# Convolving two blocks in idle PSUM banks, a spare bank for two up tiles, and a softmax in smaller parts

## The reference

```python
# 1. causal convolution over 7 steps with weights per row and head (8 heads of 24 features)
w = exp(weight_gen - max(weight_gen, axis=-1)); w = w / (sum(w, axis=-1) + 1e-9)
out[b, s, h, g] = sum over k of w[b, s, h, k] * x_pad[b, s + k, h, g]      # x_pad: 6 zero rows in front
# 2. gated layer, 1536 hidden features
g = x @ w_gate; x = (g / (1 + exp(-g)) * (x @ w_val)) @ w_out
# 3. plain layer, 2048 hidden features
h = x @ w_in;   x = (h * clip(h + 3, 0, 6) / 6) @ w_out
```

## Time and profile before

| what | value |
|---|---|
| span, instructions | 1206.4 us, 26191 |
| TensorE matmul busy | 1189.2 us (99%) |
| VectorE busy | 882.4 us (73%) |
| ScalarE busy | 631.2 us (52%) |
| GpSimd busy | 41.8 us (3%), all of it in the first 96 us |
| chain that ended last | TensorE 91%, VectorE 6%, ScalarE 2% |
| granted TensorE clock, mean | 0.998 of full speed |

### The profile page before, as it was taken

The page is one execution under the profiler, slowest core; times in us unless marked ns, Lnnn a source line. Parts: engine busy times, 40 slices in busy tenths (PEclk is TensorE's granted clock), DMA queues, the critical chain, the costliest instruction groups (busy, mean ns, idle before and its releaser), DMA issues.

```text
span 1206.4 us, 26191 instructions
## 1 busy us (share of the span) xinstructions
PE 1189.2 (99%) x10412; PEld 1022.8 (85%) x10412; DVE 882.4 (73%) x1336; ACT 631.2 (52%) x1096; POOL 41.8 (3%) x38
## 2 busy tenths in 40 slices
PE   8999999999999999999999999999999999999998
PEld 6769789889888988988889898888989888898877
DVE  6987796776868677686776868677696776864565
ACT  5455636455464554636546364553636556364555
POOL 5331000000000000000000000000000000000000
PEclk9999999999999999999999999999999999999999
DMA  8312002020200203002030110202002020100000
GB/s 228 108 48 64 1 15 65 1 77 1 60 19 8 71 2 77 2 13 66 1 77 1 34 45 5 73 1 77 1 11 67 2 77 1 27 18 5 10 10 18
DMA packets 77779, 44.86 MB, mean 37 GB/s; under 512 B 54264, under 2 KB 69880, under 8 KB 77556
## 3 DMA queue, kind: packets, MB, share of 16 engines
q1 hardware_dynamic: 77684, 43.41, 13.5%
HBM read 31.58 MB, written 11.80 MB: 36 GB/s over the span
## 4 chain that ended last, share of the span: by engine, by line
PE 91%; DVE 6%; ACT 2%; issue 1%; DMA 0%; ACTq 0%; DVEq 0%
PE up_pair L920 34%; PE acc L935 23%; PE up_pair L926 17%; PE acc L942 16%; DVE hid_lo L767 1%; DVE hidden L762 1%; DVE prod_even L637 1%; DVE hidden L759 1%; DVE sum_even L641 0%; ACT hidden L510 0%; DVE prod_odd L637 0%; DVE taps L315 0%; DVE tap_max L623 0%; ACT hidden L508 0%; PE acc L1223 0%
## 5 line engine op out<-in xcount | busy, mean ns | idle before, releaser
L920 PE MATMUL up_pair<-in_hi,up_hi 64*128 64x512 f32 x1280 | 350.6, 393 | 9.3 <-DVE hidden L759 5.3
L920 PE MATMUL up_pair<-in_hi,up_lo 64*128 64x512 f32 x1280 | 347.2, 387 | 0.0
L920 PE MATMUL up_pair<-in_lo,up_hi 64*128 64x512 f32 x1280 | 347.1, 387 | 0.0
L935 PE MATMUL acc<-hid_hi,dn_hi 64*128 64x512 f32 x872 | 337.3, 387 | 0.3 <-DVE hid_lo L767 0.3
L942 PE MATMUL acc<-hid_hi,dn_tail 64*128 64x512 f32 x872 | 337.3, 387 | 0.1
L935 PE MATMUL acc<-hid_lo,dn_hi 64*128 64x512 f32 x872 | 336.8, 386 | 0.0
L942 PE MATMUL acc<-hid_lo,dn_tail 64*128 64x512 f32 x872 | 336.7, 386 | 0.0
L935 PE MATMUL acc<-hid_hi,dn_lo 64*128 64x512 f32 x872 | 336.7, 386 | 0.0
L762 DVE SCALAR_TENSOR_TENSOR hidden<-hidden,up_pair 128x512 f32<-128x512 f32 x256 | 175.9, 688 | 198.6 <-ACT hidden L510 198.6
L767 DVE TENSOR_TENSOR hid_lo<-hidden,hid_hi 128x512 fp32r<-128x512 f32 x448 | 310.6, 693 | 1.0
L510 ACT ACTIVATE hidden<-up_pair,half_col 128x512 f32<-128x512 f32 x256 | 176.4, 689 | 225.2 <-DVE hid_lo L767 162.1
(11 more groups left out here) (120 smaller groups left out, 1387.4 us busy)
## 6 DMA issues: line engine op xcount, KB each, us to landing
window<-in_x_dram SPq DMA_DIRECT2D x14, 960.0 KB
out_dram<-out_rows SPq DMA_DIRECT2D x360, 16.0 KB, 1.5
turned_dram<-in_turned SPq DMA_DIRECT2D x56, 96.0 KB, 4.6
out_main<-turned_dram SPq DMA_DIRECT2D x14, 256.0 KB, 2.9
in_tail<-turned_dram SPq DMA_DIRECT2D x28, 128.0 KB, 3.1
stage<-in_moe_w_out_dram SPq DMA_DIRECT2D x7, 384.0 KB, 3.4
taps<-in_weight_gen_dram SPq DMA_DIRECT2D x1, 1456.0 KB, 8.2
stage<-in_moe_w_in_dram SPq DMA_DIRECT2D x4, 256.0 KB, 3.9
```

The costliest lines, as they stand in the source:

```text
L920: return nc.tensor.matmul(dst[:, :], w[lane[half], col:col + P], a[lane[half], :], start=first and product == 0, stop=False)
L935: return nc.tensor.matmul(acc[y][0], w[lane[half], k, :], a[lane[half], n % RING, :], start=half == LOW and product == 0 and k == 0, stop= ...
```

## The change

- Blocks 1 and 2 are convolved by `early_conv_op`: the normalised weights and the running sum z lie in the idle banks `acc_pair[2]`, and the sum is added up in order. Every product and sum then has one operand in SBUF and one in PSUM. The operations still number 17.
- For block 1 operations 0 to 4 (the last of them the first product, which needs the window of block 1) run ahead of period 0, and the twelve others take the slots of `conv1_gaps`, ten of them slot 0. For block 2 they take `conv2_gaps`, eleven of the 17 being slot 0, up to tile 11; the transpose `turn_input(2)` moves to slot 0 of plain tile 0.
- In blocks 0 and 1 gated tile 2 is put into `acc_pair[1]` or `acc_pair[2]` (`free_pair`), so it doesn't wait for the product of tile 0, and tile 4 waits for tile 0 instead of tile 2. The first down product of block 0 waits for the product of tile 2.
- Weight pieces 16 to 23 are copied behind gated tiles 4 to 11 of period 1 instead of 0 to 7.
- The eight softmax operations of the rest take slot 0 of plain tiles 1 to 8 (n = 13 to 20), one each. The exponentials are four operations at n = 18 to 21, and a tiny exponential at n = 17 brings the table in.
- The input copies and low parts of the next block come one tile later.
- Two pairs of spare matmuls come ahead of the last transposed product set, one pair behind it (`keep_warm`).

```diff
@@ -104,7 +104,7 @@
...
-    turns = [(0, n) for n in range(PIECES1 + STAGES - OWN)] + [(1, n) for n in range(N1)]
+    turns = [(0, n) for n in range(PIECES1 + STAGES - OWN)] + [(1, n) for n in range(LAG, N1)]
     splits_at = {turn: q for q, turn in zip(range(OWN, PIECES), turns)}
@@ -144,8 +144,8 @@
...
         half_col = sb("half_col", [P, 1])
-        warm = sb("warm", [P, 2])
-        spare = sb("spare", [P, 79])
+        warm = sb("warm", [P, 3])
+        spare = sb("spare", [P, 78])
@@ -188,6 +188,12 @@
...
         first_sets = [(6,), (5,), (4,), (3, 2), (1, 0)]
+        def free_pair(i, n):
+            if n == 2 and isinstance(i, int) and i < 2:
+                return acc_pair[i + 1]
+            return up_pair[n % 2]
@@ -415,11 +421,11 @@
...
                 load_piece(q)
-            sp.wait_ge(s_conv, LAST_PRODUCT)
+            sp.wait_ge(s_conv, LAST_PRODUCT + 1)
             load_window(2)
...
                 load_piece(q)
-            sp.wait_ge(s_conv, CONV_OPS + LAST_PRODUCT)
+            sp.wait_ge(s_conv, CONV_OPS + LAST_PRODUCT + 1)
             load_window(3)
@@ -505,7 +511,7 @@
...
                 if n < N1:
-                    nc.scalar.activation(buf, up_bank[2 * (n % 2)][:, :], ACT.Silu).then_inc(s_bent, 1)
+                    nc.scalar.activation(buf, free_pair(i, n)[:, 0, :], ACT.Silu).then_inc(s_bent, 1)
                 else:
@@ -516,9 +522,9 @@
...
-            def exponentials_rest(half):
-                act.wait_ge(s_shifted, 2 + (half + 1) * HALF)
-                exponentials(rest[half * HALF] * K, rest[(half + 1) * HALF] * K)
+            def exponentials_rest(part):
+                act.wait_ge(s_shifted, 3 + part)
+                exponentials(rest[part] * K, rest[part + 1] * K)
@@ -564,8 +570,10 @@
...
                         round_hi(i, n - 1)
-                    if fixed(i, 1) and n in (N1 + 11, N1 + 13):
-                        exponentials_rest((n - N1 - 11) // 2)
+                    if fixed(i, 1) and n == N1 + 5:
+                        nc.scalar.activation(warm[:, 2:3], half_col[:, :], ACT.Exp)
+                    if fixed(i, 1) and N1 + 6 <= n < N1 + 6 + PARTS:
+                        exponentials_rest(n - N1 - 6)
                     if isinstance(i, int) and (i, n) in splits_at:
@@ -575,9 +583,9 @@
...
                         take_sum2(i - 2)
-                    if n == N1 + 9 and has_next and not fixed(i, 0):
+                    if n == N1 + 10 and has_next and not fixed(i, 0):
                         input1_hi(i + 1)
-                    if n == N1 + 10 and has_next and not fixed(i, 0):
+                    if n == N1 + 11 and has_next and not fixed(i, 0):
                         input1_tail_hi(i + 1)
@@ -640,10 +648,8 @@
...
-            def normalise(w, k, done, base):
-                if k > 0:
-                    dve.wait_ge(done, base + k)
+            def normalise(w, k):
                 if k == 0:
@@ -696,16 +702,49 @@
...
+            def early_conv_op(b, k):
+                base = (b - 1) * CONV_OPS
+                w = tap_weights(b)
+                z, zt = sums_in(acc_pair[2]), taps_in_banks(acc_pair[2])
+                def early_product(j, dst):
+                    return nc.vector.tensor_tensor(dst, by_step_pair(window[:, j * D:(j + STEPS) * D]),
+                                                   zt[:, :, :, j:j + 1].to_broadcast([P, 2, HEADS // 2, G]), ALU.mult)
+                wait(dve, s_conv, base + (k if k < 5 or k % 2 == 0 else k - 1))
+                if k < 3:
+                    last = normalise(w, k)
+                elif k == 3:
+                    if b == 2:
+                        dve.wait_ge(s_hidden, N1 + 3)
+                    last = nc.vector.tensor_tensor(zt, w.rearrange("p (a h) k -> p a h k", a=2),
+                                                   denom[:, :].rearrange("p (a h) -> p a h", a=2).unsqueeze(3)
+                                                   .to_broadcast([P, 2, HEADS // 2, K]), ALU.mult)
+                elif k == 4:
+                    dve.wait_ge(s_window, b * (2 * B * 16))
+                    dve.wait_ge(s_in_banks, b)
+                    last = early_product(0, z)
+                else:
+                    j = (k - 3) // 2
+                    prod = (prod_even, prod_odd)[j % 2]
+                    if k % 2 == 1:
+                        last = early_product(j, by_step_pair(prod[:, :]))
+                    else:
+                        to = z if k < CONV_OPS - 1 else by_step_pair(sum_even[:, :])
+                        last = nc.vector.tensor_tensor(to, z, by_step_pair(prod[:, :]), ALU.add)
+                last.then_inc(s_conv, 1)
             def conv_op(b, k):
...
                 if k < 4:
-                    last = normalise(w, k, s_conv, base)
+                    if k > 0:
+                        dve.wait_ge(s_conv, base + k)
+                    last = normalise(w, k)
                 elif k == 4:
                     dve.wait_ge(s_conv, base + 4)
-                    if fixed(b, 1):
-                        dve.wait_ge(s_in_banks, 1)
                     dve.wait_ge(s_window, b * (2 * B * 16))
@@ -756,7 +795,7 @@
...
                     dve.wait_ge(s_val, i * N1 + n + 1)
-                    nc.vector.tensor_tensor(buf, buf, up_bank[2 * (n % 2) + 1][:, :], ALU.mult).then_inc(s_hidden, 1)
+                    nc.vector.tensor_tensor(buf, buf, free_pair(i, n)[:, 1, :], ALU.mult).then_inc(s_hidden, 1)
                 else:
@@ -817,26 +856,35 @@
...
+            conv1_gaps = [(0, 0), (1, 0), (3, 0), (4, 0), (5, 0), (6, 0), (7, 0), (7, 1), (8, 0), (9, 0), (9, 1), (10, 0)]
+            conv2_gaps = [(0, 0), (0, 1), (1, 0), (2, 0), (3, 0), (4, 0), (4, 1), (5, 0), (6, 0), (6, 1), (7, 0), (8, 0),
+                          (8, 1), (9, 0), (9, 1), (N1 - 1, 0), (N1 - 1, 1), (N1, 0)]
             def between(i, n, slot):
...
                 if fixed(i, 0):
-                    k = n if n < LAG else LAG + 2 * (n - LAG) + slot
-                    if (n >= LAG or slot == 0) and k < CONV_OPS:
-                        if k == 0:
-                            dve.wait_ge(s_exp, 2)
-                        conv_op(1, k)
+                    if (n, slot) in conv1_gaps:
+                        early_conv_op(1, conv1_gaps.index((n, slot)) + CONV_OPS - len(conv1_gaps))
                     return
-                if fixed(i, 1) and N1 + 6 <= n < N1 + 6 + HALF:
-                    if (n, slot) == (N1 + 6, 0):
+                if fixed(i, 1) and slot == 0 and N1 < n <= N1 + 2 * PARTS:
+                    part = (n - N1 - 1) // 2
+                    if n == N1 + 1:
                         dve.wait_ge(s_taps_rest, 16)
-                    part = 2 * (n - N1 - 6) + slot
-                    shift_max(rest[part], rest[part + 1])
-                elif fixed(i, 1) and N1 + 6 + HALF <= n < N1 + 6 + PARTS:
-                    part = 2 * (n - N1 - 6 - HALF) + slot
-                    dve.wait_ge(s_tap_max, 3 + part)
-                    shift_sub(rest[part], rest[part + 1]).then_inc(s_shifted, 1)
+                    if (n - N1) % 2 == 1:
+                        shift_max(rest[part], rest[part + 1])
+                    else:
+                        dve.wait_ge(s_tap_max, 3 + part)
+                        shift_sub(rest[part], rest[part + 1]).then_inc(s_shifted, 1)
+                    return
+                if fixed(i, 1) and (n, slot) in conv2_gaps:
+                    k = conv2_gaps.index((n, slot))
+                    if k < CONV_OPS:
+                        early_conv_op(2, k)
+                    else:
+                        turn_input(2)
+                    return
                 if (n, slot) in out_gaps:
@@ -845,18 +893,18 @@
...
                             turn_output_tail(i - 2)
-                elif (n, slot) in conv_gaps and has_next:
+                elif (n, slot) in conv_gaps and has_next and not fixed(i, 1):
                     k = conv_gaps.index((n, slot))
-                    if k == 0 and not fixed(i, 1):
-                        dve.wait_ge(s_exp, 4)
+                    if k == 0:
+                        dve.wait_ge(s_exp, 2 + PARTS)
                     if k < CONV_OPS:
...
                     input2_lo(i - 1, slot)
-                elif n in (N1 + 10, N1 + 11) and slot == 1 and has_next:
-                    input1_lo(i + 1, n - N1 - 10)
+                elif n in (N1 + 11, N1 + 12) and slot == 1 and has_next:
+                    input1_lo(i + 1, n - N1 - 11)
                 elif n == N1 + 5 and slot == 1 and not fixed(i, BLOCKS):
@@ -892,6 +940,9 @@
...
             input1_lo_banks(0)
+            dve.wait_ge(s_exp, 2)
+            for k in range(CONV_OPS - len(conv1_gaps)):
+                early_conv_op(1, k)
             periods(dve, period)
@@ -950,14 +1001,20 @@
...
                     wait(pe, s_mid, i)
+                if y == 1 and k == 0 and i == 0:
+                    pe.wait_ge(s_hidden, 3)
                 if y == 2 and k == 0 and i == 1:
```

(16 more changed lines are left out.)

## The result

The changed kernel takes 1212.67 us (median of 8 runs, 1211.02 to 1213.59) against 1207.88 us for the kernel before: ratio 1.0035, interval 1.0024 to 1.0045. It is slower by 4.8 us. (The 1208.63 of the kernel before that the prediction starts from was the median of its first three runs; 1207.88 is the median of all eight.) The profiled execution took 1213.14 us and has a span of 1211.3 us, 4.9 more than before.

A forecast was written before the change was run, and what follows sets the result against it. A chain (bend, product, slot 0, hid_lo, next bend but one buffer) sets the pace, not a busy share. 2.7 us in period 0 plus 1.6 to period 2 make 4.3 us, giving 1212.9 us (+0.36%), range 1205 to 1216.

The forecast's parts named there:

- Part 1: Opening of period 0: product 0 waits behind the window's reader, starts at 24.0 instead of 22.50; TensorE 2.0 us later.
- the window's landing: Opening: arrival of block 1's 945 KB window, taken as 23.1 us, with bounds 20.0 and 23.2.
- Part 2: Opening: TensorE's clock falls to half while it waits for product 1, costing 1.6 us (bounds 0 and 3.2).
- the hole: Opening: TensorE stands waiting for product 1 until 26.2, for 4.6 us, or 3.2 if the clock falls as before.
- Parts 3 and 4: Gated tiles: period 0 ends 2.7 us late; period 1 adds 0.3 by its last input low part, 1.7 by bend 13.
- the collision: Gated tiles: hid_lo, both inputs in SBUF, waits for GpSimd's weight subtraction: 1.19 us with a down piece, 0.89 with a main.
- the moved weights give back what the PSUM form wins: Gated tiles of period 1: with later weight pieces the second input low part starts at 101.5 against 101.20, 0.3 late.
- Part 5: Plain tiles: eight tiles of 2.87 us instead of four, against two long exponentials and table load; period 2 starts 1.6 late.
- drain: ScalarE's table load: the Trainium skill's extra 1.38 us per switch, not seen in the trace; would cost 1.1 us more.
- the window lands in time: Rival, opening: the 945 KB are in by 20 us, removing 3.6 us: 1209.3, no change; chance 0.20.
- hid_lo goes ahead of GpSimd: Rival, gated tiles: hid_lo wins the 0.1 us margin, down and main tiles fall, saving 7.1 us: 1205.8; chance 0.20.
- the clock stays up in the new hole: Rival, opening: clock stays full or recovers at once, saving 1.6 us: 1211.3, still slower; chance 0.15.

The follow-up runs named there:

- item 2: Changed kernel with the softmax laid out as before (both slots of plain tiles 6 to 9, two long exponentials): 1212.46 us, ratio 1.0031.
- item 3: Changed kernel with the same eight softmax operations in slot 1, behind hid_lo, instead of slot 0: 1207.37 us, ratio 0.9992.
- Item 4: Changed kernel with the convolution of blocks 1 and 2 in slot 1 where a tile has a weight piece: 1205.4 us, ratio 0.9978.
- item 6: Changed kernel with weight pieces 16 to 23 back behind gated tiles 0 to 7 of period 1: 1211.94 us, ratio 1.0026.
- item 9: Changed kernel without the six spare matmuls: 1212.67 us, ratio 1.0034.
- item 10: Kernel before with only the spare bank for tile 2 in blocks 0 and 1 added: 1208.25 us, ratio 1.0001.
- item 8: Changed kernel with block 1's window reader at tile 2, convolution and softmax moved to slot 1, tile 2 finished before tile 3 begins: 1195.31 us, ratio 0.9892.
- item 1: Changed kernel with operation 4 of block 1, first reader of the window, moved from ahead of period 0 to tile 2: 1208.59 us, ratio 1.0003.

## Why the prediction was right

The time was forecast at 1212.9 and is 1212.67; the direction and the mechanisms hold. That the two numbers agree to 0.2 us is partly luck. The loss was forecast at 4.3 us and is 4.8, and the median of the kernel before, to which the forecast added it, has come down from 1208.63 to 1207.88. Inside the sum, errors of opposite sign cancelled in part.

- **Part 1, the opening: right in kind, 1.7 us short.** Product 0 came at 25.72, not 24.0. The mis-sized term is the window's landing: 23.1 by a neighbouring DMA, and here VectorE waited until 24.85. In items 2, 3, 4, 6 and 9 it waited until 24.25, 24.19, 24.69, 24.57 and 23.12: it varies by 1.7 us. The spare bank bought nothing, as forecast (item 10); item 8 fits the reason given, the order in `up_alone`.
- **Part 2, the clock: right.** It fell in the hole. From product 1's end (27.9) to bend 2 went 4.0 us, where before it was 2.5: 1.5 against a forecast of 1.6. The hole was 5.86 us long where 4.6 was forecast, and it ended at half clock in every profile that has it (5.86 us here, 4.14 in item 9). Not foreseen is the second stretch of low clock at 106.3, behind TensorE's wait ahead of plain tile 0. From the last input low part to bend 13 went 7.8 us in the change and in item 2, which has it too; in items 1 and 3, without it, 6.9. So it cost 0.9. The waits ahead of it were as long in all four (2.45 to 2.49 us), so this too is chance from execution to execution.
- **Parts 3 and 4, the gated tiles: right.** A down tile took 3.88 us (33.83 to 37.71) for 4.00 forecast. hid_lo stayed the collision, at 1.74 (forecast 1.87). Item 4 takes the collision away and gains 7.3 us. At the last input low part of period 1 the kernel was 3.1 us late for 3.0 forecast. That the moved weights give back what the PSUM form wins is argued from this: moved back alone (item 6) they gave 0.7 us, which is not clear of noise.
- **Part 5, the softmax: right.** Bends were 2.86 to 2.90 apart for eight tiles, and the exponentials and the table load were hidden. No drain shows: the load starts as the rounding before it ends (124.76), and the tiny exponential 1.30 us later. Item 2 shows the exchange to be even; item 3 shows what slot 1 would have given.
- **How the errors cancelled.** At bend 2 the kernel was 1.6 us later than forecast, by the window's landing. The tiles of period 0 from bend 4 on gave back 0.7 (23.5 for 24.2), and those of period 1 another 0.6 up to the last input low part, where only 0.1 was left. The second stretch of low clock, not foreseen, brought the lateness back to 0.8 at bend 13, and the plain tiles kept it (38.6 us, as forecast, and 0.7 at bend 0 of period 2). So the forecast was near in the gated tiles by errors of opposite sign, and in the plain tiles by its own sum.
- **The rivals.** That the window lands in time and that hid_lo goes ahead of GpSimd did not happen, but both prices came out near when the edits made them happen: items 1 (4.1 for 3.6) and 4 (7.3 for 7.1 by the medians, 6.3 between the profiles, with some 0.9 of clock in it). That the clock stays up in the new hole didn't happen in any profile that has the hole.

## What to carry to other kernels

Before work is put into an engine's idle slot, ask whether the instruction that the next engine waits for stands behind that slot; the same operation cost 0.83 us in front of it and nothing behind it. Moving operands to a memory that doesn't collide helps only those operations: look for the one that still collides and is on the chain. A wait put ahead of an in-order engine's first urgent instruction charges everything behind it with the latest landing of a transfer, which no one needed to know while its reader came late.

## What had not been expected of the hardware

The granted clock behind the same instructions differs from execution to execution (0.50 or 1.00 at 16.6 us, and low until after 22 us in one profile). For product 1 it made 0.9 us (22.62 in item 10, 23.50 before) and, in the third profile of the kernel before, about 2.1 (25.63 against 22.62, less the 0.9 of the late window of block 0). TensorE's wait of 2.45 to 2.49 us ahead of plain tile 0 was followed by half clock in three profiles (the change, items 2 and 9) and by full clock in two (items 1 and 3). VectorE's wait for a transfer of 945 KB ended between 23.1 and 24.9 us in six profiles, with its issue within 0.7 us.
